# Thresholded attention and two MLPs: exp ahead of the roundings on ScalarE, eight value splits on VectorE, MLP2's weight splits in another order

## What is computed

```python
scores = scale * np.matmul(q, k.transpose(0, 1, 3, 2))
thresh = np.max(scores, axis=-1, keepdims=True) - tau
scores = np.where(scores >= thresh, scores, -1000000000.0)
attn = softmax(scores)                       # sum + 1e-9 below the line
x = np.matmul(attn, v)                       # -> (2304, 512)
h = x @ w_in;  x = (h / (1 + exp(-1.702 * h))) @ w_out      # MLP1
h = x @ w_in2; x = (h * tanh(log1p(exp(min(h, 20))))) @ w_out2   # MLP2
```

## Time and profile before

| | us |
|---|---|
| median of 3 runs | 1233.15 (1231.0 to 1237.72) |
| the profiled execution | 1233.13 |
| its span, first to last instruction | 1231.2 |
| TensorE busy | 1120.8 (91%) |
| VectorE busy | 778.0 (63%) |
| ScalarE busy | 738.2 (60%) |
| GpSimd busy | 338.8 (28%) |

### The profile page before, as it was taken

How to read it: one execution, slowest core, us unless ns; L and a number is a source line. 1 busy time by engine, 2 the same in 40 slices (tenths; PEclk the granted TensorE clock), 3 DMA queues, 4 the chain that set the end, 5 groups by cost and what they waited for, 6 DMA issues and landing times.

```text
span 1231.2 us, 19607 instructions
## 1 busy us (share of the span) xinstructions
PE 1120.8 (91%) x7472; PEld 1060.3 (86%) x7472; DVE 778.0 (63%) x1396; ACT 738.2 (60%) x1008; POOL 338.8 (28%) x662
## 2 busy tenths in 40 slices
PE   4658898899988999998989999999899999999998
PEld 4648888888987889888989999998798989989897
DVE  4877886787876877787867833456543444434343
ACT  4677775677666766767767622356545555444553
POOL 5975453444344443444543300000000000000000
PEclk9787998999999989999999999999899999999999
DMA  7632123222223322233222110530000000101000
GB/s 238 203 94 60 51 67 91 69 75 85 63 66 88 85 70 81 57 85 84 70 85 69 26 41 18 180 124 31 26 26 26 26 26 12 41 1 32 21 27 26
DMA packets 95118, 81.48 MB, mean 66 GB/s; under 512 B 47665, under 2 KB 80433, under 8 KB 95025
## 3 DMA queue, kind: packets, MB, share of 16 engines
q1 hardware_dynamic: 95024, 80.24, 22.5%
HBM read 66.06 MB, written 14.16 MB: 65 GB/s over the span
## 4 chain that ended last, share of the span: by engine, by line
PE 59%; DVE 15%; ACT 11%; DMA 7%; issue 5%; POOL 2%; SPq 0%; ACTq 0%; DVEq 0%
PE ps_s L670 15%; PE ps_r L565 12%; PE ps_r L693 8%; PE ps_r L586 7%; DMA k_ll_raw<-in_k 6%; PE ps_t L693 4%; PE ps_s L431 4%; PE ps_t L443 3%; PE ps_t L586 3%; PE ps_r L456 3%; DVE e_buf L496 3%; DVE pt_lo L509 2%; ACT e_buf L471 2%; ACT e_buf L464 2%; ACT pt_hi L476 2%
## 5 line engine op out<-in xcount | busy, mean ns | idle before, releaser
L565 PE MATMUL ps_r<-x_hi,wi_lo 128*128 128x256 f32 x544 | 160.9, 296 | 1.6 <-DVE g_lo_raw L604 1.1
L443 PE MATMUL ps_t<-ident,e_buf 128*128 128x128 f32 x720 | 112.6, 291 | 53.8 <-DVE pt_lo L509 41.0
L496 DVE SCALAR_TENSOR_TENSOR e_buf<-ps_s,thr,e_buf 128x576 f32<-128x576 f32 x144 | 117.1, 813 | 62.9 <-ACT e_buf L464 59.7
L565 PE MATMUL ps_r<-x_lo,wi_hi 128*128 128x256 f32 x544 | 155.9, 287 | 0.0
L565 PE MATMUL ps_r<-x_hi,wi_hi 128*128 128x256 f32 x544 | 155.8, 286 | 0.0
L476 ACT CAST pt_hi<-ps_t 128x640 fp32r<-128x640 f32 x144 | 99.9, 694 | 86.0 <-PE ps_t L443 83.5
L737 DVE COPY hidden<-ps_s 128x768 f32<-128x768 f32 x48 | 45.6, 956 | 164.4 <-PE ps_s L670 164.4
L509 DVE TENSOR_TENSOR pt_lo<-ps_t,pt_hi 128x640 fp32r<-128x640 f32 x144 | 118.1, 820 | 49.6 <-ACT pt_hi L476 47.6
L526 POOL TENSOR_SCALAR thr<-neg_max,tau_sb 128x1 f32<-128x1 f32 x144 | 59.1, 411 | 327.8 <-DVE neg_max L488 326.0
L586 PE MATMUL ps_r<-g_hi,wo_lo 128*128 128x256 f32 x464 | 137.1, 295 | 7.9 <-DVE g_lo L615 3.8
L443 PEld LDWEIGHTS ps_t<-ident,e_buf 128*128 128x128 f32 x720 | 88.4, 150 | 63.0 <-ACT e_buf L471 28.3
(11 more groups left out here) (95 smaller groups left out, 3113.8 us busy)
## 6 DMA issues: line engine op xcount, KB each, us to landing
k_ll_raw<-in_k SPq DMA_DIRECT2D x64, 288.0 KB, 2.8
v_st_raw<-in_v SPq DMA_DIRECT2D x64, 160.0 KB, 3.0
wi_lo_raw<-in_moe_w_in SPq DMA_DIRECT2D x16, 512.0 KB, 5.4
wo_lo_raw<-in_moe_w_out SPq DMA_DIRECT2D x16, 512.0 KB, 5.7
q_raw<-in_q SPq DMA_DIRECT2D x32, 192.0 KB, 2.9
x_lo_raw<-x_scratch SPq DMA_DIRECT2D x9, 512.0 KB, 4.1
x_scratch<-y_acc SPq DMA_DIRECT2D x9, 512.0 KB, 3.5
x_lo_raw<-x_scratch SPq DMA_DIRECT2D x6, 768.0 KB, 4.6
```

The source lines that it names most:

```text
L443: mm = pe.transpose(t_flat[:, j * P:(j + 1) * P], e_buf[n % 3][:, j * P:(j + 1) * P], ident[:, :])
L496: dve.scalar_tensor_tensor(out=e, in0=scores(n), scalar=thr[:, c], in1=e, op0=ALU.is_ge, op1=ALU.mult, accum_out=row_sum[:, c]).then_inc(s ...
L565: mm = pe.matmul(bank[:, part * CH:(part + 1) * CH], wi[w][:, k, f * P:(f + 1) * P], x[:, k, :], start=t == 0, stop=t == 3 * KT - 1)
```

## The change

On ScalarE a slot's list gets another order: behind tanh, pt_hi and g_hi now come the product's copy (slots from 18 on), pt_hi where it had stood late, norm(n-1) and exp(n), and only then the roundings of keys, queries, values, weights and x. The v_lo of the eight uses of the front, which are made in slots 2 to 16, goes from GpSimd to VectorE, there at the end of the next slot; the others stay. W2_WITH goes on over the last two downs, with four pieces that had followed group 0, and ScalarE's rounding of the other four follows groups 0 and 1 in place of 1 and 2. VectorE's list is read one group later, so that its splits keep their places, but for the first four, which now stand around the last y.

```diff
+        def dve_v_lo(dve, u):
+            v = v_st[u % 2]
+            dve.wait_ge(s["v_hi"], u + 1)
+            dve.tensor_tensor(v[:, :, D:P], v_raw[u % 2][:, :, D:P], v[:, :, 0:D].bitcast(F32),
+                              ALU.subtract).then_inc(s["v_lo_first"], 1)
...
-            pe.wait_ge(s["v_lo"], u + 1)
+            if u < H:
+                pe.wait_ge(s["v_lo_first"], u + 1)
+            else:
+                pe.wait_ge(s["v_lo"], u - H + 1)
...
-                   enumerate(((0, 0), (0, 1), (1, 2), (2, 4), (4, 6), (6, 8)))}
-        W2_BEHIND = {0: W2_ORDER[8:12], 1: W2_ORDER[12:14], 2: W2_ORDER[14:16]}
+                   enumerate(((0, 0), (0, 1), (1, 2), (2, 4), (4, 6), (6, 8), (8, 10), (10, 12)))}
+        W2_BEHIND = {0: W2_ORDER[12:14], 1: W2_ORDER[14:16]}
...
                 for pair in ups_at(n - 2):
                     act_g_hi(act, pair)
+                if n >= FRONT + 2 and n - 3 in GROUP_AT:
+                    act_pv(act, GROUP_AT[n - 3])
+                if not turn_first and 0 <= n - 2 < N:
+                    act_p_hi(act, n - 2)
+                if FRONT <= n - 1 < N:
+                    act_norm(act, n - 1)
+                if 0 <= n < N:
+                    act_exp(act, n)
                 if n < FRONT + 2 and n - 4 in GROUP_AT:
                     act_pv(act, GROUP_AT[n - 4])
                 for u in K_PREP.get(n, []):
                     act_k_hi(act, u)
                 for u in Q_PREP.get(n, []):
                     act_q_hi(act, u)
-                if n >= FRONT + 2 and n - 3 in GROUP_AT:
-                    act_pv(act, GROUP_AT[n - 3])
                 for u in V_PREP.get(n, []):
                     act_v_hi(act, u)
                 if n in W_SLOT:
                     act_w_hi(act, 0, W_SLOT[n])
-                if not turn_first and 0 <= n - 2 < N:
-                    act_p_hi(act, n - 2)
                 if n in X_HI:
                     act_x_hi(act, X_HI[n])
-                if FRONT <= n - 1 < N:
-                    act_norm(act, n - 1)
-                if 0 <= n < N:
-                    act_exp(act, n)
...
+                for u in V_PREP.get(n - 1, []):
+                    if u < H:
+                        dve_v_lo(dve, u)
                 if n - 1 in W_SLOT:
                     dve_w_lo(dve, W_SLOT[n - 1])
...
-                for c in W2_BEHIND.get(g, []):
+                for c in W2_BEHIND.get(g - 1, []):
                     dve_w2_lo(dve, c)
...
                 for u in V_PREP.get(n, []):
-                    pool_v_lo(pool, u)
+                    if u >= H:
+                        pool_v_lo(pool, u)
```

2 lines of the change are left out of this document (1 added, 1 removed).

## The result

| | before | after |
|---|---|---|
| median of 4 runs, us | 1232.42 (1231.0 to 1237.72) | 1186.34 (1183.23 to 1186.64) |
| the profiled execution, us | 1233.13 | 1183.23 |
| its span, us | 1231.2 | 1180.6 |
| TensorE busy, us | 1120.8 (91%) | 1097.8 (93%) |

The ratio is 0.9613, with a 95% interval of 0.9580 to 0.9646. The direction was right. The size of term 2 was not, and term 3 shows no gain at all.

The account below looks back on a forecast made before the run. TensorE was taken as busy for 1120.8 of 1231.2 us, its idle time lying in three places. Terms of 9.1, 17 and 6.5 us sum to 32.6, giving 1200.5 us, range 1188 to 1217.

Parts of the forecast that it names:

- term 2: Mixed stage, attention with MLP1 pieces: ScalarE's new order shortens TensorE's waits; 17 us, bounds 6 and 25.
- term 3: First 107 us: GpSimd spared v_lo gives 2.5 us, ScalarE's new order the rest; 6.5 us, bounds 0 and 10.
- Term 1: MLP2's start: earlier weight roundings remove TensorE waits and a half-clock projection; 9.1 us, bounds 5 to 9.4.
- hand count of 22 us: Mixed stage: expected savings in waits added slot by slot, 22 us, before the cut to 17.
- The ceiling is 48.2 - 19 = 29 us.: Mixed stage: most that could be gained, 48.2 us of waits less a 19 us floor no ScalarE order gives back.
- The half-clock turns and matmuls behind the long waits [...] may give 2 us more: Mixed stage: possible extra 2 us from work at half clock, counted only in the upper bound.
- The discount of 5 us: Mixed stage: 22 us cut to 17, as shifts were counted against one engine only and VectorE is 78% busy.
- VectorE [...] is nearly the bound itself: First 107 us: with v_lo, VectorE goes from about 6.9 to 7.4 us in two slots.
- three upper bounds: Largest gains allowed: 9.4 us at MLP2's start, 25 in the mixed stage, 10 in the first 107 us.
- The lock decides early: First 107 us: v_lo on VectorE and GpSimd stall each other, zero or +2 us, 1208; chance 0.08 shared with another rival.
- Mostly a trade: Moved roundings meet the next slot's pt_hi and tanh; mixed stage keeps 6 us, front 3, time 1215; chance 0.24.
- Slower: ScalarE waits for max, then rounds in front of pt_hi, making it late; TensorE loses 32 us, 1256; chance 0.02.

Follow-up runs that it names:

- e1: The kernel before with the new order of MLP2's weight splits alone; 1225.0 us, ratio 0.9937.
- e12: The kernel before with 40 extra matmuls, results unused, in TensorE's wait ahead of chunk 1 of MLP2; 1233.5 us, ratio 0.9980.
- e4: The kernel before with ScalarE's new order from slot 18 on, the front as it was; 1190.72 us, ratio 0.9652.
- e5: The changed kernel with the eight v_lo of the front back on GpSimd; 1178.77 us, ratio 0.9552.
- e16: The changed kernel with the eight v_lo on VectorE right behind max, not at the slot's end; 1176.96 us, ratio 0.9540.
- e13: The changed kernel with the front's eight v_lo subtractions left out, ScalarE copying the values once more instead; 1178.33 us, ratio 0.9546.
- e10: The kernel before with ScalarE's new order alone, and pt_hi made twice in slots from 24 on with an MLP piece; 1202.99 us, ratio 0.9736.

## Why the prediction was right or wrong

**Term 1, MLP2's start: right.** I gave 9.1 us, and it is 9.0, with 0.5 us left ahead of chunk 1. Since e1 alone gives 9.0 too, it owes nothing to the rest. The clock's part, which I had inferred from one row, was confirmed by e12, at 2.7 us for 3.0.

**Term 2, the mixed stage: mechanism right, size wrong, 41.7 us for 17.** The steps on single slots hold: I had 4.1 us for slot 131 (4.15), 2.2 each for 41, 77 and 113 (2.0, 2.2, 2.6), and 2.0 for slot 69 (1.9). The whole hand count of 22 us is what TensorE's listed waits lost, 57.4 to 34.7. Three steps failed.
- "The ceiling is 48.2 - 19 = 29 us." I took it from the matmuls' waits. The weight loads', which stand in the same profile, were 71.7 us, and fell by 31.6. The matmuls' busy time is modelled and covers part of such a wait: TensorE's busy time in the stage fell by 18 us with the same matmuls (from 540.0 to 522.3), some 9 of it such covered waits and some 8 clock.
- "The half-clock turns and matmuls behind the long waits [...] may give 2 us more". I priced one turn at 0.6 us. Whole stretches of 2 to 5 us go with the long waits, and they were worth some 8 us.
- "Since each shift was counted against one other engine only [...] I take 17." The discount of 5 us was for roundings that would meet the next slot's work. They don't: ScalarE still idled ahead of pt_hi, 45 us in the stage where it had been 64, so the roundings end before it is due. The listed waits lost the 22 us whole.

Added up, from 17 to 41.7 us: the discount was 5.7 us too much, the weight loads' waits fell by 8.9 us more than the matmuls', the clock gave some 8, and some 2 are open.

**Term 3, the first 107 us: wrong, 0 for 6.5.** Two of its parts came about as said: the new order gives 5.4 us up to mask(24), 2.7 by mask(16) and 2.6 behind it (3.3 in e4), where I had said 1 and 3; with 3 us between executions no more than that can be said of either. The third, 2.5 us from the relief of GpSimd, failed: "On VectorE [...] I take 0.5 [...] 0.35 to 0.4 net in two slots". The split does take 0.48 us. But I costed it by busy time and not by its place, ahead of the next mask, where it cost 6 us at mask(24) against e5 and 7.6 in the median. Nor does GpSimd's relief count at mask(24) where v_lo stands well: in e16 two slots of GpSimd take 7.7 us over norm(6) to norm(14), for 8.0 in e5, and TensorE waits for pt_lo instead. "VectorE [...] is nearly the bound itself" was the sentence to price. e16 is 0.3 us from e5 at mask(24), and e13 0.4.

**The rivals.** "The lock decides early" had the right stage and nearly the right size (zero or +2), and part of the mechanism, "VectorE becomes the bound"; but it named the engines' sharing, and e16, with v_lo on the same engine, shows that the place decides. "Mostly a trade" said that exp would wait for max in place of rounding. It does (8.4 to 19.1 us), and it costs nothing, because that wait ends as soon as max does, and a rounding doesn't. "Slower" needed pt_hi to come late behind roundings, and ScalarE's idle time ahead of it says that it doesn't; only the 67 us of e10 bring such waits.

**The range.** Its low end, 1188, is what the three upper bounds give together (9.4 + 25 + 10, 1188.8). Term 2 alone was 17 us above its upper bound, because the bound rested on the wrong ledger. That the time came within 1.7 us of the range is luck: term 3 missed by 6.5 us the other way.
